# One fp32 attention-and-MLP kernel: the first steps in another order, the squares of x moved from GpSimd to ScalarE

## The reference: what is computed

```
attn = softmax(where(mask, q @ k.T / 8, -1e9)) @ v       # x: [2304, 512]
xn   = x / sqrt(mean(x*x) + 1e-6) * rms_g
g    = xn @ w_gate
x2   = (g * sigmoid(g) * (xn @ w_val)) @ w_out
h    = x2 @ w_in
y    = (h * sigmoid(1.702 * h)) @ w_out2
```

## Time and profile before

| | |
|---|---|
| median of 3 runs | 904.08 us (903.5 to 904.87) |
| the profiled execution | 904.1 us, of which its span is 901.6 us |
| TensorE busy | 889.1 us, 99% of the span |
| VectorE, ScalarE, GpSimd busy | 60%, 44%, 9% |

### The profile page before, as it was taken

The page is one execution under the profiler, slowest core; times in us unless marked ns, Lnnn a source line. Parts: engine busy times, 40 slices in busy tenths (PEclk is TensorE's granted clock), DMA queues, the critical chain, the costliest instruction groups (busy, mean ns, idle before and its releaser), DMA issues.

```text
span 901.6 us, 14706 instructions
## 1 busy us (share of the span) xinstructions
PE 889.1 (99%) x5372; PEld 771.3 (86%) x5372; DVE 539.6 (60%) x1256; ACT 398.5 (44%) x941; POOL 82.2 (9%) x114
## 2 busy tenths in 40 slices
PE   8899999999999999999999999999999999999998
PEld 7799888888888888888888899999999999999997
DVE  6886634334333343433336578887788788867663
ACT  5676333343333423334123354545464554545442
POOL 6234001030010300113000000000000000000000
PEclk9999999999999999999999999999999999999999
DMA  7672111102111021100500222121432122241201
GB/s 253 205 218 96 51 51 51 50 24 74 51 50 51 24 73 51 51 25 1 186 1 24 94 96 69 60 81 47 164 117 94 48 74 67 67 145 47 71 24 70
DMA packets 41078, 69.75 MB, mean 77 GB/s; under 512 B 3632, under 2 KB 13872, under 8 KB 41008
## 3 DMA queue, kind: packets, MB, share of 16 engines
q1 hardware_dynamic: 39600, 67.12, 23.0%
q10 hardware_dynamic: 1408, 1.70, 0.6%
HBM read 59.38 MB, written 9.44 MB: 76 GB/s over the span
## 4 chain that ended last, share of the span: by engine, by line
PE 94%; DVE 3%; ACT 2%; issue 1%; POOL 1%; POOLq 0%; ACTq 0%; DVEq 0%
PE ps L631 16%; PE ps L633 15%; PE ps L632 15%; PE ps L825 7%; PE ps L826 7%; PE ps L824 7%; PE ps L767 7%; PE ps L763 7%; PE ps L765 6%; PE ps L612 2%; PE ps L584 2%; PE ps L598 2%; DVE w_all L1197 1%; ACT prob L867 0%; DVE sig L1235 0%
## 5 line engine op out<-in xcount | busy, mean ns | idle before, releaser
L631 PE MATMUL ps<-x_hi,w_all 128*128 128x512 f32 (+1 forms) x480 | 179.4, 374 | 0.2 <-DVE x_lo L1137 0.2
L633 PE MATMUL ps<-x_lo,w_all 128*128 128x512 f32 (+1 forms) x480 | 176.7, 368 | 0.0
L632 PE MATMUL ps<-x_hi,w_all 128*128 128x512 f32 (+1 forms) x480 | 176.7, 368 | 0.0
L826 PE MATMUL ps<-w2out,hB 128*128 128x512 f32 x288 | 113.0, 392 | 0.0
L825 PE MATMUL ps<-w2out,hB 128*128 128x512 f32 x288 | 112.9, 392 | 0.0
L824 PE MATMUL ps<-w2out,hB 128*128 128x512 f32 x288 | 112.0, 389 | 0.0
L631 PEld LDWEIGHTS ps<-x_hi,w_all 128*128 128x128 f32 x480 | 90.4, 188 | 18.4 <-issue 3.0
L633 PEld LDWEIGHTS ps<-x_lo,w_all 128*128 128x128 f32 x480 | 90.4, 188 | 15.3
L632 PEld LDWEIGHTS ps<-x_hi,w_all 128*128 128x128 f32 x480 | 90.4, 188 | 14.6
L1235 DVE SCALAR_TENSOR_TENSOR sig<-sig,ps 128x512 f32<-128x512 f32 x48 | 32.9, 686 | 107.1 <-ACT sig L981 107.1
L631 PE MATMUL ps<-h_hi,w_all 128*128 128x512 f32 (+1 forms) x240 | 90.4, 376 | 1.8 <-DVE hid L1244 1.6
(11 more groups left out here) (144 smaller groups left out, 1557.0 us busy)
## 6 DMA issues: line engine op xcount, KB each, us to landing
wstage<-in_w_b SPq DMA_DIRECT2D x48, 512.0 KB, 3.7
wstage<-in_w_a SPq DMA_DIRECT2D x36, 256.0 KB, 3.2
vwin<-in_v_win SPq DMA_DIRECT2D x32, 256.0 KB, 3.9
kwin<-in_k_t SPq DMA_DIRECT2D x32, 160.0 KB, 3.3
x2raw<-x_scratch SPq DMA_DIRECT2D x3, 1536.0 KB, 7.5
out_dram<-yB SPq DMA_DIRECT2D x18, 256.0 KB, 4.4
qtok<-in_q_t SPq DMA_DIRECT2D x34, 128.0 KB, 2.6
x_scratch<-wstage SPq DMA_DIRECT2D x3, 1024.0 KB, 4.2
```

The source lines that it names most:

```text
L631: pe.matmul(out_, w[:, 0, cols], xh, start=first, stop=False, **flags)
L632: pe.matmul(out_, w[:, 1, cols], xh, start=False, stop=False, **flags)
L633: return pe.matmul(out_, w[:, 0, cols], xl, start=False, stop=last, **flags)
L826: ins = pe.matmul(y, hB_of(g, chunk, 1)[:, rows], w[:, 0, chunk, :], start=False, stop=last)
```

## The change

**First steps.** TensorE's order becomes transposes 2, `probs_by_v(1)`, transposes 3, `probs_by_v(2)`, `probs_by_v(3)`, then the four parts of the first chunk; one pair of `keep_busy` matmuls goes. The weight pieces (0,1), (1,1) and (2,1) are cast by ScalarE and no longer by GpSimd, ScalarE's squares of steps 0 to 3 come after all four `first_x_hi`, and VectorE splits the pieces in the order of the new list `FIRST_SPLITS`. SP loads q, k and v of steps 4 and 5 ahead of pieces (2,1) and (2,2), and waits for the sixth split, (0,2), before it issues (2,2). The semaphore of the probability copies is split in two, by engine.

**Gates scaled first.** In tile 0 `scale_gate(1)` comes right after `scale_gate(0)`, into a place of its own (the second half of `ss`), and tanh of chunk 1 right after tanh of chunk 0. The splits of (2,1) and (1,2) move into chunk 0, and that of (4,0) moves from before `silu_A(0, 2)` to behind the second normalisation of that chunk.

**Squares.** ScalarE makes them (`square_x`), behind `hid_hi_A` in chunks 4, 6 and 8 and behind the tanh in chunk 10; GpSimd only adds (`add_square`), one addition for each step but every fourth.

```diff
+        FIRST_SPLITS = ((0, 0), (0, 1), (1, 0), (1, 1), (2, 0), (0, 2), (2, 1), (1, 2), (2, 2))
...
+        CASTS_BY_ACT = ((0, 1), (1, 1), (2, 0), (2, 1)) + tuple((c, m) for c in range(3, CA) for m in range(2))
...
-            for m in range(3):
-                load_wA(2, m)
+            load_wA(2, 0)
             for s in (EARLY, EARLY + 1):
                 load_step_qk(s)
+            load_wA(2, 1)
             for s in (EARLY, EARLY + 1):
                 load_step_v(s)
+            load_wA(2, 2)
...
-                nc.gpsimd.tensor_tensor(sq[:, :], x, x, ALU.mult).then_inc(squares_done, 1)
-                pool.wait_ge(squares_done, done + 2 * c)
-                nc.gpsimd.tensor_tensor(part, part, sq[:, :], ALU.add).then_inc(squares_done, 1)
+                pool.wait_ge(squares_made, s - EARLY + 1)
+                wait(pool, squares_done, SQ * (s // PAIRS - 1) + c - 1)
+                nc.gpsimd.tensor_tensor(part, part, (sq_odd if c % 2 else sq)[:, :], ALU.add).then_inc(squares_done, 1)
...
-            keep_busy(4, 2)
             probs_by_v(2)
-            transpose_probs(3)
-            first_chunk_part(0)
             probs_by_v(3)
-            for d in range(1, DC):
+            for d in range(DC):
                 first_chunk_part(d)
...
+            def square_x(s):
+                t, c, at_ = home_of(s)
+                act.wait_ge(o_evacuated, s - EARLY + 1)
+                if c == 0:
+                    wait(act, sumsq_done, t)
+                    wait(act, squares_done, SQ * (s // PAIRS - 1))
+                else:
+                    wait(act, squares_done, SQ * (s // PAIRS - 1) + max(c - 2, 0))
+                to = ss[:, at_:at_ + GT] if c == 0 else (sq_odd if c % 2 else sq)[:, :]
+                nc.scalar.activation(to, xT[:, c, at_:at_ + GT], ACT.Square).then_inc(squares_made, 1)
...
-                    tanh_A(t, c)
-                    if c == SUMSQ_AT and t + 1 < NA:
-                        sum_hi(t + 1)
+                    if (t, c) != (0, 1):
+                        tanh_A(t, c)
+                    if (t, c) == (0, 0):
+                        tanh_A(0, 1)
...
+                    if multiplied is not None and c == SUMSQ_AT:
+                        square_x(multiplied)
+                        square_x(multiplied + 1)
+                        sum_hi(t + 1)
                     hid_hi_A(t, c)
+                    if multiplied is not None and c < SUMSQ_AT:
+                        square_x(multiplied)
+                        square_x(multiplied + 1)
...
-                    if t == 0:
+                    if t == 0 and c != 1:
                         scale_gate(c)
+                    if t == 0 and c == 0:
+                        scale_gate(1)
+                        weights_lo_A(2, 1)
...
-                    if split is not None and c > 0:
+                    if split is not None and c > 0 and c != 2:
                         weights_lo_A(split, 0)
...
+                    if split is not None and c == 2:
+                        weights_lo_A(split, 0)
```

More of the change, by code:

```diff
@@ L137, in fused_attention_mlps, with scaled_of, silu_of @@
         gsc = sig[:, GT:2 * GT]
+        def scaled_of(c):
+            return ss[:, GT:2 * GT] if c == 1 else gsc
+        def silu_of(t, c):
+            return sq[:, :] if (t, c) == (0, 1) else sig[:, 0:TILES_A[t][1]]
         def gate_bank(t, c):
@@ L255, in wait, with wait_probT @@
                 eng.wait_ge(s, value)
+        def wait_probT(eng, n):
+            if n <= 2:
+                wait(eng, first_probT_ready, n)
+            else:
+                eng.wait_ge(probT_ready, n - 2)
         def slotA(c):
@@ L261, in raw @@
             return wstage[:, (3 * u + m) * DM:(3 * u + m + 1) * DM]
+        FIRST_SPLITS = ((0, 0), (0, 1), (1, 0), (1, 1), (2, 0), (0, 2), (2, 1), (1, 2), (2, 2))
         def splitsA(c, m):
-            return 3 * c + m + 1
+            return FIRST_SPLITS.index((c, m)) + 1 if c < 3 else 3 * c + m + 1
+        CASTS_BY_ACT = ((0, 1), (1, 1), (2, 0), (2, 1)) + tuple((c, m) for c in range(3, CA) for m in range(2))
+        CASTS_BY_POOL = ((0, 0), (1, 0), (0, 2), (1, 2)) + tuple((c, 2) for c in range(2, CA))
         def cast_by_act(c, m):
-            return (c, m) == (2, 0) or (c > 2 and m < 2)
+            return (c, m) in CASTS_BY_ACT
         def casts_so_far(by_act, c, m):
-            return sum(cast_by_act(*at_) == by_act for at_ in itertools.product(range(CA), range(3)) if at_ <= (c, m))
+            return (CASTS_BY_ACT if by_act else CASTS_BY_POOL).index((c, m)) + 1
         A11, A12, A22, S1, S2, S3, S4 = range(COMBOS)
@@ L553, in _ @@
                         if multiplied is not None:
-                            squares(multiplied + i)
+                            add_square(multiplied + i)
                     if t == 0 and c + 3 < CA:
@@ L591, in transpose_probs @@
                 if s < EARLY:
-                    wait(pe, probT_ready, s - 1)
+                    wait_probT(pe, s - 1)
                 else:
@@ L959, in _ @@
             first_x_hi(0)
+            weights_hi_by_act(0, 1)
+            copy_probT(2)
             first_x_hi(1)
-            copy_probT(2)
-            first_square(0)
             copy_probT(3)
-            first_square(1)
             first_x_hi(2)
-            first_square(2)
             first_x_hi(3)
+            for s in range(EARLY):
+                first_square(s)
+            weights_hi_by_act(1, 1)
             nc.scalar.preload_act_table_set(LN_SET)
-            first_square(3)
             weights_hi_by_act(2, 0)
+            weights_hi_by_act(2, 1)
             act.wait_ge(consts_ready, 1)
@@ L979, in tanh_A @@
                     act.wait_ge(gate_done, n + 1)
-                wait(act, hidA_made, n)
-                nc.scalar.activation(sig[:, 0:w], gsc[:, :] if t == 0 else gate_of(t, c),
+                wait(act, hidA_made, n if (t, c) != (0, 1) else 0)
+                nc.scalar.activation(silu_of(t, c), scaled_of(c) if t == 0 else gate_of(t, c),
                                      ACT.Tanh, scale=0.5).then_inc(sigA_ready, 1)
@@ L1234, in silu_A @@
                 dve.wait_ge(sigA_ready, n + 1)
-                nc.vector.scalar_tensor_tensor(out=sig[:, 0:w], in0=sig[:, 0:w], scalar=1.0,
-                                               in1=gsc[:, :] if t == 0 else gate_of(t, c),
+                nc.vector.scalar_tensor_tensor(out=silu_of(t, c), in0=silu_of(t, c), scalar=1.0,
+                                               in1=scaled_of(c) if t == 0 else gate_of(t, c),
                                                op0=ALU.add, op1=ALU.mult).then_inc(siluA_done, 1)
@@ L1293, in _ @@
                         normalise(scored + 1)
+                    if split is not None and c == 2:
+                        weights_lo_A(split, 0)
                     if split is not None and c > 0:
                         weights_lo_A(split, 1)
+                    if t == 0 and c == 0:
+                        weights_lo_A(1, 2)
                     hid_lo_A(t, c)
```

51 lines of the change are left out of this document (22 added, 29 removed).

## The result

The kernel after takes 905.58 us (904.98 to 906.76, 22 runs), the kernel before beside it 904.14. The ratio is 1.0018, interval 1.0012 to 1.0024: slower by 1.44 us, where 0.4 us faster was forecast. The time lies inside the stated range of 902.0 to 905.7, near its slow end, but on the wrong side of the kernel before. The profiled execution took 905.2 us with a span of 903.3, against 904.1 and 901.6.

The account below looks back on a forecast made before the run. TensorE, busy 889.1 of 901.6 us, was taken as the bound, its waits early in tile 0 behind VectorE. Sum: 904.1 - 1.9 (start) + 0.7 (chunk 10) + 0.8 (chunks 4, 6, 8) = 903.7 us, range 902.0 to 905.7.

Parts of the forecast that it names:

- the start: Tile 0 up to chunk 4: new first steps and the moved split of (4,0) gain 1.9 us; bounds 1.0 and 2.7.
- chunks 4 to 8: Tile 0, chunks 4, 6 and 8: GpSimd's additions and cast slow VectorE's run of splits, 0.8 us lost.
- chunk 10: Tile 0: squares behind ScalarE's tanh delay the sum of squares, 0.7 us lost; bounds 0.3 and 1.1.
- The step that failed: Chunks 4, 6 and 8: GpSimd work slows VectorE's instructions only partly, two additions and a cast costing about 1.0 us.
- rival 2: Chunks 6 and 8: GpSimd and VectorE exclude each other strictly, VectorE loses 2.0 and not 1.0, 905.5 us; chance 0.12.
- of some 0.5 each: Expected TensorE waits at `probs_by_v` of steps 8 and 10, in the profile after.
- Nothing more: First projection: scaling gates first gains nothing further, as the gate's 0.33 and the split of (1,2) cancel.
- Rival 3: Start: piece (2,2) lands late, delaying the first projection, 906.8 us; decides from a landing of about 3.5 us; chance 0.09.
- Rival 1: Additions end up beside PSUM-reading VectorE instructions, GpSimd gives back nothing, the start wins 2.7: 901.7 us; chance 0.20.

Follow-up runs that it names:

- casts_by_act: all_early with GpSimd's casts of pieces (3,2) and (5,2) made by ScalarE: 901.87 us, 0.9974 to 0.9991 of before.
- all_early: The kernel after with ScalarE's squares right behind the copies of x in chunks 4, 6, 8 and 10: 902.36 us, 0.9975 to 0.9992 of before.
- c10_early: The kernel after with only chunk 10's two squares moved ahead of the tanh: 904.37 us, 0.9997 to 1.0015 of before.
- start_alone: The kernel after with GpSimd squaring and adding as before, so only first steps and gates changed: 903.59 us, 0.999 to 1.0008 of before.

## Why the prediction was wrong

The landmarks put a size on each term. Forecast and measured at the same places: the start -1.9 and -0.96, chunks 4 to 8 +0.8 and +1.69, chunk 10 +0.7 and +0.95. That is -0.4 against +1.68, with the span at +1.7.

**The step that failed** is the one behind the earlier trace rows: "1.09 against 0.69 is less than a whole wait". From it I priced an overlap at 0.4 and gave strict exclusion a chance of 0.12. But a split that starts while a cast is running sees only the rest of the cast. In the earlier trace rows the cast starts at 46.90 and in the earlier trace rows the split at 47.42, half a microsecond later. With a cast of 1.07 that leaves 0.55 to wait, some 0.45 without the tails, and 0.40 was measured. The cast's 1.07 was itself a wait: alone a cast takes 0.61, and this one started under the normalisation, which the addition before it (46.20, 0.74) had held:

```profile
46.46 1.04 DVE L1129 TENSOR_TENSOR prob<-prob,rrec 128x512 f32<-128x512 f32 x1
```

So the rows fitted exclusion in turns, and I took one of them as evidence against. The rule that rival 2 rests on, in the Trainium skill, "SBUF — State Buffer", section "Who interferes with whom", agrees with the pairs of instructions shown above, but for the overlap of some 0.1 at a turn. What I read as an average slowdown is turns. A GpSimd instruction in the middle of VectorE's run costs about three quarters of its own length (1.51 for some 2.0 in chunk 7, 0.97 for 1.3 in chunk 5), and I had charged half.

**Chunks 4, 6 and 8** were mis-sized by this step. The places and the instructions were right. Of the waits "of some 0.5 each" that of `probs_by_v(10)` was right with 0.47, and that of `probs_by_v(8)` is 1.00. In chunk 7 VectorE loses 1.51, halfway between the 1.0 of the forecast and the 2.0 of rival 2. The 0.5 more is found in the wait of 1.00. In chunk 5, 0.2 was to be won and 0.19 was lost, since its one addition and the cast hold VectorE for 0.97 (48.52 to 51.02, against 1.53). Rival 2's time of 905.5 is close to the result partly by chance. Its 1.8 us above the forecast was too much for these chunks, and the rest of the difference came from the start.

**The start** fell short by as much, 0.94, and in the trace by the same contention. At the first projection 0.79 of 1.05 came. The gate and the split of (1,2) were to cancel there; the split (25.30) fell almost wholly into the wait for ScalarE's cast, and what took back the gate's 0.33 was GpSimd's cast of (2,2), beside which `hid_lo_A` of chunk 0 took 0.83 (25.90). "Nothing more" was right by luck. Then the cast of (3,2) held `hid_lo_A` at 29.28 for 0.41 more, and the cast of (5,2), once the split of (4,0) was out of its way, held the silu at 34.31 for 0.41. The chain adds up: 0.79 - 0.41 + 1.02 - 0.41 = 0.99 at the transposes of step 5, measured 0.98. Here 1.02 is the split of (4,0) by its pace, from 34.68 in the earlier trace rows to the silu behind it at 35.70. The prediction took that length as saved. Where the contention was, another instruction now stands, so only 0.6 of it was. The copies behind `scale_gate(3)` start at 39.44, where 38.4 was forecast, and `probs_by_v(4)` follows 0.7 later as worked out. The 0.96 lies just under the lower bound of 1.0, beside which contention was named, though of two splits.

This account is of one execution of each kernel. The two other kernels with the old start have the gate of chunk 4 at 43.07 and 43.10, so of the 0.96 up to 0.18 belongs to the half clock of before. That the casts in chunks 1 and 2 cost time is borne out by casts_by_act, 0.6 by the medians. That the holds make up all of the shortfall is read from the traces alone.

**Chunk 10** was right in mechanism and a quarter short. The second addition starts 0.88 behind the first and not 0.7, and the first 0.05 later than forecast. Undone, it gives 1.3 by the spans, near the 1.48 of TensorE's waits: the 0.95, and the 0.53 that before also waited.

**The rest.** Tiles 1 to 4 and the second MLP cost nothing, as forecast (818.4 us behind the sum of chunk 10 in both). Rival 3 didn't happen: piece (2,2), issued at 22.56, landed 2.9 us later, under the 3.5 from which it decides. Rival 1 is what all_early reaches by another order. The half clock of the earlier trace rows is absent from the profiled execution, whose granted clock is 1.00 at 38 to 39 us.

## What to carry to other kernels

Ask of each instruction moved to or within GpSimd what VectorE does at that moment, and when both work in SBUF, charge it at most of its length (three quarters here). VectorE's row maxima and scaled gates, which read PSUM, stood beside it unharmed. Place such work by time and not by quantity: 18 us less GpSimd work made this kernel slower, and the same additions placed under exponentials made it faster. When an instruction beside another takes longer, compare the starts before calling the slowdown partial.

## What was unexpected of the hardware

The stretch of half clock is no property of a place in the program, nor of the kernel. The profiled execution of before has it at 38 us, that of c10_early too, that of all_early at 30 to 32 us; in those of after and start_alone it is absent. All engines of all_early and of c10_early:

```profile
30.00:32.00 2.00, 2.00 (x12) 2.00 (x11) 2.00 (x14) 0.89 (x3) 0.59 (x1) 0.50 0.88 294
```

```profile
38.00:39.00 1.00, 1.00 (x6) 1.00 (x6) 1.00 (x3) 0.00 (x0) 0.00 (x0) 0.50 0.63 113
```

A granted clock of 0.50 is the 1.2 GHz level. In both, TensorE is busy throughout the window. The stretch shows in an execution's mean granted clock: the profiled ones that have it stand at 0.998, start_alone, which lacks it, at 1.00. Of the 33 runs of the kernel before in one batch, 21 stand at 0.998 and 9 at 1.00, so it comes and goes between executions of one program.

It cost next to nothing here: those 21 runs have a median span of 901.9 and those 9 of 901.7. (Two runs at 0.996 took 902.9 and 903.9; no trace of such a run is at hand.) Why one stretch costs so little, two traces show. In the kernel after `probs_by_v(4)` waits 1.40 for its copies and starts 3.49 us behind the transposes of step 5 (40.15 and 36.66). In c10_early, the same program up to there, the half clock fills that wait, and it starts 3.53 behind them (36.80), without a wait:

```profile
40.33 1.15 PE L623 MATMUL ps<-probT,vwin 128*64 128x64 f32 x32
```

What sets its place, and whether it comes, stays open.
